# Three pairs of PSUM banks for the first round of an attention scan, and outputs of the second stream copied head by head

## The chip, the cores and the metric

The kernel runs on one core of one Trainium2 chip. The metric is the device time of one execution in microseconds (us); lower is better. Engines are named as in the profile: PE is TensorE (PEld its weight loads), DVE is VectorE, ACT is ScalarE, POOL is GpSimd and SP is SyncE, which here only issues transfers. SPq and ACTq are transfers issued from those engines' queues.

## The reference, cut to what matters

```python
def _attn_ref(r, k, v, w, u):                    # B 4, H 8, S 768, D 48
    state = zeros(B, H, D, D)
    for t in range(S):
        y[:, :, t] = r_t . (state + (u * k_t) v_t^T)
        state = w_t[:, :, :, None] * state + k_t v_t^T
x = attn.transpose(0, 2, 1, 3).reshape(B * S, H * D)     # 3072 tokens x 384
x = ((x @ w_a) * (x @ w_b)) @ w_out                      # d_ff 1536, "gated"
h = x @ w_in;  g = max(h, 0) + alpha * min(h, 0)         # d_ff 2048, "leaky"
out = g @ w_out2
```

All of it is float32. In the two feed-forward layers each factor is split in a high and a low part, and three products (high by high, high by low, low by high) are summed: lines 166 to 168 of the helper `three_products`.

## The kernel before, in words

**The scan.** Queries r, keys k and decays w lie with channels on partitions. A pair of heads is stacked at partitions 0 and 64 (48 channels each, `ROWS` = 112 rows in all), and a *unit* is such a pair in one batch. A round, called `n` or `duo` in the code, handles four units over half of the sequence (384 tokens each); they form two *streams* `j` = 0, 1 of two units. Eight rounds (`DUOS`) make the whole. Inside blocks of 64 tokens the decays are unrolled by doubling: a *leaf* step and then *levels* 1 to 5. Before level p the queries (`step_r`) and the keys (`step_k`) of each stream are multiplied by products of decays over 2^(p-1) tokens, which `products_of_w` makes; then 24 small matmuls a stream (`level`, line 696; 48 records of PE in the trace) write scores of both heads to two PSUM banks, and DVE merges them under a mask into `a_sb` (`merge_level`, line 948, one instruction a head). The leaf scores are merged by `merge_leaf` (line 938). Level 5 is copied, not merged (`copy_last_level`, one head by ACT, one by DVE). Then the keys are multiplied a last time (`last_step_k`), turned by PE (`turn_keys`, line 711), copied by ACT (`copy_kt`), multiplied with the values (`key_values`, line 725), carried through the blocks as states by DVE (`carry_states`, lines 971 and 979), and the outputs are summed: `weighted_values` (line 740) and `state_products` (line 756).

A round has 11 phases. Round 0 stands ahead of everything else and runs alone. From phase 1 of round 1 on, each phase is a slot in the loop over `g` of the gated layer (8 tiles of 384 tokens by 12 column blocks of `w_a` and `w_b`): in an iteration PE does `up_a(g)`, `down(g-1)`, `up_b(g)`, and then a phase of the scan. The leaky layer follows, without scan work.

**PSUM.** There are eight banks: `products` has five of them (numbers 0 to 4), `acc[0..2]` one each. Bank 4 is where the gated layer has its `a` product. In round 0 the gated layer doesn't run yet. The banks of a level are

```python
def level_bank(phase, hd):
    return BANK * (2 * (phase % 2) + hd)
```

so levels alternate between banks 2, 3 (odd levels) and 0, 1 (even ones), and `level` waits on PE for the merges of the level two before (`merged`). The keys of stream j are turned into banks 2j and 2j + 1, and so `turn_keys` waits for the merges of level 4, and for stream 1 for the copies of level 5 too.

**The order of the work** is written out by hand, for each engine a list, and is in order on each. In round 0 the queries and the last key step run on POOL, the other key steps and the merges on DVE; DVE's list for round 0 stands line by line at the end of its block. SP issues in its order: keys, queries and decays of round 0; the first weights (`load_piece`); the values of stream 0 and 1 (`load_v`); the queries of round 1 (`load_r`), each after the values of its own stream have landed; the keys of round 1 (`load_k`) once each stream's keys are turned; more weights; and the moves below.

**Outputs and moves.** `output_parts` lists what ACT copies out of PSUM as high parts (`copy_outputs`) and DVE subtracts for the low parts (`lower_outputs`, line 1021): stream 0 in four parts of 192 columns, stream 1 in two parts of 384 columns, both of 112 rows, where rows 48 to 63 are filler. The gated layer's input needs 128 rows: the filler rows get the fourth 16-channel pieces of a unit, which `move_rows` transfers out of `f_y` (lines 346, six of 48 KB each, `KT` = 3 by two row groups). For the first of three groups q the move waits for stream 0's parts alone, for the others for all six, since a later copy would overwrite what was moved. PE's `wait_x` asks for part 3 at kt = 0 and for all parts at kt > 0, and for the move of that kt. In round 0 ACT issues two of the six moves.

**Weights** of the gated layer come in 36 pieces through three staging buffers: SP loads, ACT splits off the high part (`split_hi`, line 138), DVE (POOL for the first five) the low part (`split_lo`, line 143). `FIRST_NEW[f]` is the first piece that is split in iteration f of the first tile; SP loads piece p + 3 into the buffer of piece p in the same iteration.

## Time and profile before

| | before |
|---|---|
| median of 3 runs | 1025.76 us (1025.4 to 1025.85) |
| profiled execution: its own time | 1024.34 us |
| its span, first to last instruction | 1022.5 us |
| PE busy | 1000.7 us, 98% of the span |
| PE idle by the stretches, 0 to 50 us | 16.8 us |
| DVE, ACT, POOL busy | 559.5, 288.7, 24.4 us |

The profiled execution lies 1.42 us under the median; 1.84 us of its time are outside of the span. A timeline row gives the start in us from the span's start, the length in us, the engine, the line, the operation with what it writes and reads, how often, and in brackets how long the engine was idle before and what ended that. The PE idle time to 50 us is the sum over stretches of length minus busy time.

### The profile page before, as it was taken

Reading aid. Unit: us, or ns where it says so; the run is one execution under the profiler, and the core shown is the slowest. Engines: PE = TensorE matmul, PEld = TensorE weight load, DVE = VectorE, ACT = ScalarE, POOL = GpSimd, SP = SyncE. Lnnn points to the kernel's source line nnn. Section 1 sums busy time; section 2 is a strip of 40 time slices with the busy share of each in tenths; the row PEclk is TensorE's granted clock in tenths of the full one; section 3 lists DMA queues with packets and bytes.
Section 4 is the critical chain, followed back from the end, with each engine's and each line's share of the span. In section 5 each row is a group of like instructions: output and inputs, shape, how many; then the busy total and the mean of one; then the engine's idle time right before and its main releaser. Section 6 shows DMA issues by size and latency. Waiting matters only on the chain.

```text
span 1022.5 us, 29089 instructions
## 1 busy us (share of the span) xinstructions
PE 1000.7 (98%) x12448; PEld 976.0 (95%) x12448; DVE 559.5 (55%) x1170; ACT 288.7 (28%) x604; POOL 24.4 (2%) x24
## 2 busy tenths in 40 slices
PE   5799999999999999999999999999999999999998
PEld 5799999999999999999999999999999999999998
DVE  7487664655656646556432437645455554545554
ACT  3435314223232242241222434222222212122212
POOL 4400000000000000000000000000000000000000
PEclk9999999999999999999999999999999999999999
DMA  6554311411213013010020313010101010101000
GB/s 159 140 156 113 87 55 30 114 29 47 69 30 91 25 30 92 15 52 25 25 60 1 114 58 124 1 47 1 47 1 47 1 46 0 46 0 47 10 15 24
DMA packets 42167, 53.01 MB, mean 52 GB/s; under 512 B 5184, under 2 KB 42048, under 8 KB 42048
## 3 DMA queue, kind: packets, MB, share of 16 engines
q1 hardware_dynamic: 40624, 51.04, 17.5%
q8 instruction: 94, 1.54, 0.6%
q10 hardware_dynamic: 1424, 0.23, 0.1%
q14 instruction: 25, 0.20, 0.1%
HBM read 39.46 MB, written 9.44 MB: 48 GB/s over the span
## 4 chain that ended last, share of the span: by engine, by line
PE 96%; DVE 1%; issue 1%; ACT 0%; DMA 0%; ACTq 0%; DVEq 0%; SPq 0%
PE products L166 18%; PE products L167 16%; PE products L168 16%; PE acc L168 12%; PE acc L166 11%; PE acc L167 11%; PE products L696 5%; PE products L711 1%; PE products L740 1%; PE products L756 1%; PE products L673 1%; PE products L725 1%; DMA x_parts<-f_y 0%; DVE k_in L931 0%; DVE a_sb L948 0%
## 5 line engine op out<-in xcount | busy, mean ns | idle before, releaser
L166 PE MATMUL products<-x_parts,weights_hi 128*128 128x384 f32 x576 | 201.0, 349 | 3.6 <-DMA x_parts<-f_y 1.5
L167 PE MATMUL products<-x_parts,weights_hi 128*128 128x384 f32 x576 | 194.2, 337 | 0.0
L168 PE MATMUL products<-x_parts,weights_lo 128*128 128x384 f32 x576 | 193.9, 337 | 0.0
L1239 DVE TENSOR_SCALAR leaky_low<-products,leaky_al 128x384 f32<-128x384 f32 x128 | 79.0, 617 | 169.6 <-PE products L168 169.5
L1099 DVE TENSOR_TENSOR g_sb<-a_g,products 128x384 f32<-128x384 f32 x96 | 53.2, 554 | 195.4 <-issue 133.1
L1186 ACT ACTIVATE leaky_g_hi<-leaky_g_sb 128x384 fp32r<-128x384 f32 x128 | 67.3, 525 | 295.0 <-DVE leaky_g_sb L1244 295.0
L514 ACT ACTIVATE g_hi<-g_sb 128x384 fp32r<-128x384 f32 x96 | 50.3, 524 | 255.0 <-DVE g_sb L1099 255.0
L166 PEld LDWEIGHTS products<-x_parts,weights_hi 128*128 128x128 f32 x576 | 108.1, 188 | 8.9 <-issue 5.0
L168 PEld LDWEIGHTS products<-x_parts,weights_lo 128*128 128x128 f32 x576 | 108.2, 188 | 0.0
L167 PEld LDWEIGHTS products<-x_parts,weights_hi 128*128 128x128 f32 x576 | 108.2, 188 | 0.0
L168 PE MATMUL acc<-g_hi,weights_lo 128*128 128x384 f32 x288 | 97.5, 338 | 0.0
L166 PE MATMUL acc<-g_hi,weights_hi 128*128 128x384 f32 x288 | 97.4, 338 | 0.0
L167 PE MATMUL acc<-g_lo,weights_hi 128*128 128x384 f32 x288 | 96.9, 336 | 0.0
L514 ACT ACTIVATE a_g<-products 128x384 f32<-128x384 f32 x96 | 47.3, 493 | 129.9 <-PE products L168 129.8
L696 PEld LDWEIGHTS products<-r_in,k_in 48*64 48x64 f32 (+1 forms) x3840 | 61.0, 139 | 13.0 <-issue 9.6
L1105 DVE TENSOR_TENSOR g_lo<-g_sb,g_hi 128x384 fp32r<-128x384 f32 x96 | 53.4, 557 | 36.3 <-ACT g_hi L514 36.1
L1226 DVE TENSOR_TENSOR leaky_g_lo<-leaky_g_sb,leaky_g_hi 128x384 fp32r<-128x384 f32 x128 | 70.3, 549 | 5.3 <-ACT leaky_g_hi L1186 4.7
L1244 DVE SCALAR_TENSOR_TENSOR leaky_g_sb<-products,leaky_low 128x384 f32<-128x384 f32 x128 | 70.4, 550 | 0.3
L696 PE MATMUL products<-r_in,k_in 48*64 48x32 f32 (+1 forms) x3840 | 65.7, 223 | 3.4 <-DVE a_sb L948 1.4
L167 PE MATMUL products<-x_parts,leaky_rest_hi 128*128 128x384 f32 x192 | 65.0, 339 | 0.0
L166 PE MATMUL products<-x_parts,leaky_rest_hi 128*128 128x384 f32 x192 | 64.9, 338 | 0.0
L168 PE MATMUL products<-x_parts,leaky_rest_lo 128*128 128x384 f32 x192 | 64.9, 338 | 0.0
(85 smaller groups left out, 1754.9 us busy)
## 6 DMA issues: line engine op xcount, KB each, us to landing
k_in<-in_k_dram SPq DMA_DIRECT2D x16, 336.0 KB, 4.2
r_in<-in_r_dram SPq DMA_DIRECT2D x16, 336.0 KB, 5.2
stage<-in_w_out_dram SPq DMA_DIRECT2D x14, 384.0 KB, 3.2
w_v<-in_v_dram SPq DMA_DIRECT2D x16, 288.0 KB, 3.8
y_dram<-x_in SPq DMA_DIRECT2D x8, 576.0 KB, 3.0
x_in<-y_dram SPq DMA_DIRECT2D x8, 576.0 KB, 4.6
out_dram<-leaky_out_sb SPq DMA_DIRECT2D x7, 576.0 KB, 3.3
stage<-in_w_dram SPq DMA_DIRECT2D x10, 336.0 KB, 3.8
```

The lines of the kernel that those rows point to most:

```text
L166: pe.matmul(out, w_hi, x_hi, start=first, stop=False)
L167: pe.matmul(out, w_hi, x_lo, start=False, stop=False)
L168: return pe.matmul(out, w_lo, x_hi, start=False, stop=last)
L514: return act.activation(out, in_, ACT.Copy)
L673: last = pe.matmul(view(tile, at + BLOCK * c, [[1, BLOCK]], BLOCK, BLOCK * par), key_blocks(k_scratch[j], hd, c, par), key_blocks(r_leaf[j ...
L696: last = pe.matmul(view(products, level_bank(phase, hd) + 32 * (CH * j + c), [[1, 32]], rows, BLOCK * par), key_blocks(k_in[j], hd, c, par ...
L1099: dve.tensor_tensor(g_sb[:, :], a_g[:, :], b_ps(g), ALU.mult).then_inc(g_ready, 1)
L1105: dve.tensor_tensor(g_lo[f % 2][:, :], g_sb[:, :], g_hi[f % 2][:, :].bitcast(F32), ALU.subtract).then_inc(g_lo_ready, 1)
L1186: return act.activation(out_, in_, ACT.Copy)
L1226: dve.tensor_tensor(self.g_lo[f % 4][:, :], self.g_sb[f % 2][:, :], self.g_hi[f % 4][:, :].bitcast(F32), ALU.subtract).then_inc(self.g_lo_ ...
L1239: dve.tensor_scalar(self.low[f % 2][:, :], h, 0.0, self.al[:, f:f + 1], ALU.min, ALU.mult).then_inc(self.low_ready, 1)
L1244: dve.scalar_tensor_tensor(self.g_sb[f % 2][:, :], h, 0.0, self.low[f % 2][:, :], ALU.max, ALU.add).then_inc(self.g_ready, 1)
```

## The change

It does five things.

1. In round 0 the levels use three pairs of banks: levels 1 and 4 have banks 2, 3, level 2 banks 0, 1, level 3 `acc[0]` and `acc[1]`, level 5 bank 4 and `acc[2]`. The keys of stream 1 are turned into `acc[0]`, `acc[1]`. PE's waits are now for merges that lie further back.
2. On DVE the key steps of a level go ahead of the merges of the levels before; the last key steps of round 0 move from POOL to DVE, and POOL waits for them before its last query steps.
3. On ACT `copy_last_level` of round 0 goes behind the copies of the turned keys.
4. SP loads the queries of round 1 after both loads of values have landed, and the second of them after the first has landed.
5. Stream 1's outputs are copied and lowered in four parts of 48 rows in every round, in place of two of 112 rows, so all six moves need stream 0's parts alone; SP issues five of them in round 0 and ACT one, ahead of the copies of stream 1. Beside this `FIRST_NEW` has one piece in iteration 1 and two in iteration 3, where there were two and one.

```diff
-OUTPUTS = 6
+OUTPUTS = 8
-FIRST_NEW = [5, 5, 7, 9, 10, 11, 13, 15, 16, 17, 18, 18, 18]
+FIRST_NEW = [5, 5, 6, 8, 10, 11, 13, 15, 16, 17, 18, 18, 18]
...
-            def level_bank(phase, hd):
-                return BANK * (2 * (phase % 2) + hd)
+            def level_ps(n, phase, hd):
+                if n == 0 and phase == 3:
+                    return acc[hd], 0
+                if n == 0 and phase == 5:
+                    return (products, 4 * BANK) if hd == 0 else (acc[2], 0)
+                return products, BANK * (2 * ((phase + (n == 0 and phase == 4)) % 2) + hd)
+
+            def keys_ps(n, j, hd):
+                return (acc[hd], 0) if n == 0 and j == 1 else (products, stream_bank(j, hd))
...
-                units_of_1 = (0, 2, hi[0:ROWS, TT:3 * TT], lo[0:ROWS, TT:3 * TT])
+                units_of_0 = [(0, ROWS, *group) for group in units_of_0]
+                units_of_1 = [(row0, D, 0, 2, hi[row0:row0 + D, TT:3 * TT], lo[row0:row0 + D, TT:3 * TT]) for row0 in (0, 64)]
...
                 def move_last_unit(n):
+                    sp.wait_ge(copied, outputs_copied(n, 3))
+                    sp.wait_ge(lowered, outputs_lowered(n, 3))
                     for q in range(KT):
-                        part = 3 if q == 0 else OUTPUTS - 1
-                        sp.wait_ge(copied, outputs_copied(n, part))
-                        sp.wait_ge(lowered, outputs_lowered(n, part))
-                        for row0 in ((0, 64) if n > 0 or q == 0 else (0,)):
+                        for row0 in ((0, 64) if n > 0 or q < KT - 1 else (0,)):
                             move_rows(sp, n, q, row0)
...
-                                if n == 0:
-                                    sp.wait_ge(v_loaded[j], 16)
+                                if n == 0 and j == 0:
+                                    sp.wait_ge(v_loaded[0], 16)
+                                    sp.wait_ge(v_loaded[1], 16)
+                                elif n == 0:
+                                    sp.wait_ge(r_loaded[2], 16)
                                 load_r(n + 1, j)
...
                         if step == 6:
-                            last_step_k(0, j)
+                            pool.wait_ge(k_last[1], 1)
...
-                    if phase == 6:
+                    if phase == 6 and n > 0:
                         copy_last_level(n)
                     elif phase == 7:
                         copy_kt(n, 0)
                         copy_kt(n, 1)
+                        if n == 0:
+                            copy_last_level(n)
                     elif phase == 10:
                         copy_outputs(n, 0)
                         if n == 0:
                             shared.split_hi(act, BETWEEN_OUTPUTS)
+                            act.wait_ge(lowered, outputs_lowered(n, 3))
+                            move_rows(act, n, KT - 1, 64)
                         copy_outputs(n, 1)
-                        if n == 0:
-                            act.wait_ge(lowered, outputs_lowered(n, OUTPUTS - 1))
-                            for q in range(1, KT):
-                                move_rows(act, n, q, 64)
...
                     h = 1 << phase
-                    if phase >= 3:
+                    if n == 0:
+                        if 2 <= phase <= 4:
+                            pe.wait_ge(merged, (merges(0, 0, 1), merges(0, 0, 3), merges(0, 1, 1))[phase - 2])
+                    elif phase >= 3:
                         pe.wait_ge(merged, merges(n, phase - 2, 1))
...
                 def turn_keys(n, j):
-                    if j == 0:
+                    if n == 0:
+                        pe.wait_ge(merged, merges(0, 2 + j, 1))
+                    elif j == 0:
                         pe.wait_ge(merged, merges(n, 4, 1))
...
                 def key_values(n, j):
                     pe.wait_ge(copied, copies(n, "keys", j, 1))
+                    if n == 0 and j == 1:
+                        pe.wait_ge(merged, merges(0, 4, 1))
...
+                step_k(0, 1, 1)
                 merge_leaf(0, 1)
-                step_k(0, 1, 1)
                 step_k(0, 0, 2)
+                step_k(0, 1, 2)
+                products_of_w(0, 0, 2, (3,))
                 merge_level(0, 0, 1)
                 merge_level(0, 1, 1)
...
```

The semaphore arithmetic (`copies`, the parts in `lower_outputs`) follows these and is left out. What the lists become on DVE in round 0 (line numbers shift: `step_k`, 931, is 947 now, `merge_level`, 948, is 965, and 1012 is `last_step_k`), from the merges of level 2 on:

```order
L948 COPY_PREDICATED a_sb<-level_mask,products 128x96x4 [waits merged,masks_loaded,products_done1] x2
L931 TENSOR_TENSOR k_in0<-k_in0,f_y 112x48x8 [waits products_done0,k_stepped0,f_done]
L948 COPY_PREDICATED a_sb<-level_mask,products 128x48x8 [waits merged,masks_loaded,products_done1]
L931 TENSOR_TENSOR k_in1<-k_in1,f_y 112x48x8 [waits products_done1,k_stepped1,f_done]
L948 COPY_PREDICATED a_sb<-level_mask,products 128x48x8 [waits merged,masks_loaded,products_done1]
L931 TENSOR_TENSOR k_in0<-k_in0,f_y 112x24x16 [waits products_done0,k_stepped0,f_done]
L948 COPY_PREDICATED a_sb<-level_mask,products 128x24x16 [waits merged,masks_loaded,products_done1]
L931 TENSOR_TENSOR k_in1<-k_in1,f_y 112x24x16 [waits products_done1,k_stepped1,f_done]
L948 COPY_PREDICATED a_sb<-level_mask,products 128x24x16 [waits merged,masks_loaded,products_done1]
```

This was before; the same engine and place with the change:

```order
L965 COPY_PREDICATED a_sb<-level_mask,products 128x96x4 [waits merged,masks_loaded,products_done1] x2
L947 TENSOR_TENSOR k_in0<-k_in0,f_y 112x24x16 [waits products_done0,k_stepped0,f_done]
L947 TENSOR_TENSOR k_in1<-k_in1,f_y 112x24x16 [waits products_done1,k_stepped1,f_done]
L965 COPY_PREDICATED a_sb<-level_mask,acc0 128x48x8 [waits merged,masks_loaded,products_done1]
L1012 TENSOR_TENSOR k_in0<-k_in0,f_y 112x12x32 [waits products_done0,k_stepped0,f_done]
L1012 TENSOR_TENSOR k_in1<-k_in1,f_y 112x12x32 [waits products_done1,k_stepped1,f_done]
L965 COPY_PREDICATED a_sb<-level_mask,acc1 128x48x8 [waits merged,masks_loaded,products_done1]
L965 COPY_PREDICATED a_sb<-level_mask,products 128x24x16 [waits merged,masks_loaded,products_done1] x2
```

The key steps of level 3 (48x8) now stand ahead of level 2's merges (96x4), and both last key steps stand between the merges of level 3.

On SP, the loads of round 1's queries and what stands around them, before:

```order
L350 DMA w_v<-in_v_dram 128x2x288 [waits k_first0,f_done,r_stepped0,staged1]
L350 DMA w_v<-in_v_dram 128x2x288 [waits k_first1,f_done,r_stepped1,staged2]
L350 DMA r_in<-in_r_dram 112x2x384 [waits v_loaded0]
L350 DMA r_in<-in_r_dram 112x2x384 [waits v_loaded1]
L350 DMA k_in<-in_k_dram 112x2x384 [waits products_done0]
L350 DMA k_in<-in_k_dram 112x2x384 [waits products_done1]
```

and with the change:

```order
L361 DMA w_v<-in_v_dram 128x2x288 [waits k_first0,f_done,r_stepped0,staged1]
L361 DMA w_v<-in_v_dram 128x2x288 [waits k_first1,f_done,r_stepped1,staged2]
L361 DMA r_in<-in_r_dram 112x2x384 [waits v_loaded1,v_loaded0]
L361 DMA r_in<-in_r_dram 112x2x384 [waits r_loaded2]
L361 DMA k_in<-in_k_dram 112x2x384 [waits products_done0]
L361 DMA k_in<-in_k_dram 112x2x384 [waits products_done1]
```

The order is the same; the two waits moved.

## Rows read from the trace of the kernel before

**Rows 1.** The page, part 1: busy us (share of the span) and instructions.
```profile
PE 1000.7 (98%) x12448; PEld 976.0 (95%) x12448; DVE 559.5 (55%) x1170; ACT 288.7 (28%) x604; POOL 24.4 (2%) x24
```
**Rows 2.** Windows: stretch, length, busy us (records) by engine, granted clock, DMA share, GB/s.
```profile
8.00:20.00 12.00, 9.38 (x326) 8.87 (x323) 10.26 (x16) 3.83 (x8) 6.57 (x6) 1.00 0.51 127
20.00:30.00 10.00, 7.22 (x285) 6.68 (x281) 7.27 (x14) 2.20 (x4) 7.58 (x9) 1.00 0.58 154
40.00:50.00 10.00, 8.15 (x204) 7.30 (x201) 4.38 (x11) 3.92 (x9) 3.66 (x2) 1.00 0.47 122
100.00:200.00 100.00, 99.78 (x1809) 95.33 (x1807) 60.51 (x143) 30.29 (x70) 0.00 (x0) 1.00 0.25 67
```
**Rows 3.** The chain of waits from 0 to 52 us: start, length, what.
```profile
28.32 2.32 issue
...
44.13 2.99 DMA x_parts<-f_y
```
**Rows 4.** Timeline of PE in round 0 and behind it.
```profile
19.01 2.79 PE L696 MATMUL products<-r_in,k_in 48*64 48x32 f32 x96 [1.36 <-DVE a_sb L948]
...
26.55 0.87 PE L696 MATMUL products<-r_in,k_in 48*32 48x32 f32 x48 [0.49 <-DVE k_in L931]
27.34 0.98 PE L711 MATMUL products<-ident,k_in 48*64 48x48 f32 x25
30.64 2.15 PE L711 MATMUL products<-ident,k_in 48*64 48x48 f32 x69 [2.32 <-issue]
...
36.23 1.53 PE L740 MATMUL products<-a_sb,w_v 64*48 64x64 f32 x48 [0.79 <-DVE state L979]
...
54.57 1.60 PE L696 MATMUL products<-r_in,k_in 48*64 48x32 f32 x96
```
**Rows 5.** DMA queues from 24 to 28 us, then from 28 to 30: packets, MB, share.
```profile
q1 hardware_dynamic: 459, 0.66, 65.0%
...
q8 instruction: 1, 0.02, 3.6%
```
**Rows 6.** Timeline of SP: the loads of round 1's queries.
```profile
24.32 1.05 SPq L350 DMA_DIRECT2D r_in<-in_r_dram  x2
```
**Rows 7.** Timeline of DVE, then POOL, in round 0.
```profile
17.11 1.85 DVE L948 COPY_PREDICATED a_sb<-level_mask,products 128x384 f32<-128x384 int32 x2
22.40 0.89 DVE L931 TENSOR_TENSOR k_in<-k_in,f_y 112x384 f32<-112x384 f32 x1
...
22.00 0.87 POOL L490 TENSOR_TENSOR r_in<-r_in,f_y 112x384 f32<-112x384 f32 x1 [0.41 <-PE products L696]
```
**Rows 8.** Timelines of PE, SP and DVE at the end of round 0.
```profile
44.84 0.42 PE L166 MATMUL products<-x_parts,weights_hi 128*128 128x384 f32 x1 [0.36 <-DMA x_parts<-f_y]
47.26 0.41 PE L166 MATMUL products<-x_parts,weights_hi 128*128 128x384 f32 x1 [1.13 <-DMA x_parts<-f_y]
...
41.80 4.24 SPq L346 DMA_DIRECT2D x_parts<-f_y  x4
...
43.03 1.02 DVE L1021 TENSOR_TENSOR x_parts<-products,x_parts 112x384 fp32r<-112x384 f32 x2 [1.31 <-ACT x_parts L514]
43.97 1.04 DVE L938 COPY_PREDICATED a_sb<-leaf_mask,products 128x384 f32<-128x384 int32 x2
```
**Rows 9.** Timelines of ACT and PE behind the outputs of round 3.
```profile
246.17 1.11 ACT L514 ACTIVATE x_parts<-products 112x192 fp32r<-112x192 f32 x3
247.23 0.49 ACT L514 ACTIVATE a_g<-products 128x384 f32<-128x384 f32 x1
...
248.62 0.33 PE L166 MATMUL products<-x_parts,weights_hi 128*128 128x384 f32 x1
```
**Rows 10.** Timelines of PE, DVE, SP and ACT in the gated layer's iterations 1 to 4.
```profile
63.03 0.41 PE L166 MATMUL products<-x_parts,weights_hi 128*128 128x384 f32 x1 [0.41 <-DVE g_sb L1099]
...
60.60 1.82 DVE L143 TENSOR_TENSOR weights_lo<-stage,weights_hi 128x768 fp32r<-128x768 f32 x2
...
67.27 3.49 SPq L133 DMA_DIRECT2D stage<-in_w_b_dram  x6
...
71.65 0.49 ACT L514 ACTIVATE a_g<-products 128x384 f32<-128x384 f32 x1 [1.40 <-PE products L168]
```

52 lines of the change are left out of this document (32 added, 20 removed).

## The prediction

> **What bounds the kernel now.** I began with the page's busy times: PE is busy for 98% of the span [rows 1]. The windows say where the missing 2% lie. From 100 to 200 us PE idles for 0.22 us; up to 50 us it idles for 16.8 us (the table above), 7.25 of them in the three stretches before 50 us [rows 2], where the granted clock reads 1.00 throughout. So only the scan's round 0 and the first iterations of the gated layer have time to give; behind them anything that the change does can only keep PE waiting. The chain of waits up to 52 us names two large single pieces [rows 3]: 2.32 us of "issue" at 28.32, and 2.99 us for a move into `x_parts` that ends at 47.13. Beside these, the levels leave small gaps of 0.4 to 1.6 us, which end with a merge or a key step of DVE [rows 4].
>
> **The gap at 28.32** stands within `turn_keys` of stream 0: 25 records of 48, then nothing, then the other 23 in one go with stream 1's 48 [rows 4]. No semaphore lies between them. What the trace has there is the DMA queues' share [rows 5]: from 24 to 28 us the DMA engines carry 0.66 MB, 65% busy, for the loads of round 1's queries, which SP issued from 24.32 on [rows 6], and no instruction packet; between 28 and 30 us there is one packet of 0.02 MB on q8, the queue of instructions. I read this as PE running out of instructions, since the fetch of the next block stood behind the query loads. The Trainium skill (Runtime: NRT & Kernel Launch, "Instruction fetch mechanics") says that instructions come in blocks of 16 KiB through a DMA queue of the engine's own, and that the cost of a block is mostly hidden; q8's packet has that size, the 2.32 us contradict "hidden" for this place. By that sentence the gap would have another cause and stay; this is the second rival.
>
> **The change, step by step.**
>
> *Loads of the queries (SP).* The first now waits for both loads of values. Stream 1's query load of before, which waited for the second load of values, was the second of the two issues [rows 6] and began near 25.05, so the first load is issued some 0.7 us later, and its packets run from about 26 instead of 25.3. PE leaves level 4 near 24.4 and needs the new block at the 26th record of `turn_keys`, 28.1. If the fetch is asked for near 25.4 it is ahead of the packets now. Gain 2.32, with 0 as the other bound. I take 2.32, since the second query load can't stand in the way: it waits for the first one's landing, near 28.7. What is queued behind it on SP are the key loads of round 1. Those are issued only once keys are turned, so they lose nothing, but the three loads now go out within about 1.5 us.
>
> *Levels (PE, DVE).* Level 3 on PE started at 19.01, released by a merge [rows 4]. Now it needs only the leaf's merges, and can start when level 2 of stream 1 ends, near 17.5: 1.5 us earlier. Little of this lives until the turn. DVE was busy for 10.26 of 12 us and 7.27 of 10 [rows 2], and it has the same instructions to do, with one key step more (0.56, from POOL) and three merges fewer (0.56 each) ahead of the first turned keys; the two merges of level 1 take 1.85 [rows 7] and now stand ahead of level 3's key steps. POOL works beside it, and a DVE step with two SBUF inputs that meets POOL's takes 0.89 instead of 0.56 [rows 7]: key steps that are released by the same matmuls as POOL's query steps meet them always. Walking the list with these lengths I get level 4 at 21.6 to 22.2, level 5 at 24.9, and the turn at 27.1 instead of 27.34. Gain 0.25; bounds -0.4 (each meeting lost) and 1.5 (level 3's lead kept).
>
> *Behind the turn.* From the break's end to `weighted_values` of stream 0 it took 5.59 us (30.64 to 36.23) [rows 4]: turned keys, ACT's copies, products, ten state steps. The same instructions stay on this path. ACT's copy of level 5, 0.97 long, leaves it and hides beside the key-value products; level 3's second merge must now be done before stream 1's keys turn, near 28.3, just in time. So `weighted_values` start near 33.7.
>
> *The next blocks of instructions.* The three loads that now leave close together are 1 MB; at the pace of before (0.66 MB in 65% of 4 us, 0.25 MB a us [rows 5]) they run from 30 to 34 while PE needs further blocks. I charge 0.2 us; bounds 0 and 0.85 (a fetch that starts only when the last key load is through).
>
> *Moves (SP, ACT, PE).* PE waited 1.13 us at 47.26 for the second group's move [rows 8], 1.29 us start to start beyond a matmul's 0.18. All moves now go out from 41.80 on, where SP's four took 4.24 including its wait for stream 1 [rows 8]; five at about 0.65 end near 45, so the second group lands near 46.4, in time. But DVE has two more subtractions of 0.47 ahead of the leaf merges, which started at 43.97 [rows 8]: the first ends near 45.9, and PE's first `w_b` product waits for it, with 45.36 as the time that it had. Of the 15 matmuls behind it the last starts near 48.45 instead of 49.26. Gain 0.8; bounds 0 (ACT's move issue, 0.7 long, holds its copies, or the fifth move is late) and 1.3. Cover for the rest: the low parts of stream 1 are wanted only at the second group.
>
> *Outputs in rounds 1 to 7.* ACT has two more copies, DVE two more subtractions (2 x 0.5, hidden: DVE is busy for 60.5 of 100 us there [rows 2]). ACT's three copies took 1.06 until `a_g` [rows 9], one of them half as long: 0.40 for a full one. So `a_g` ends at 247.72 + 0.8 = 248.5, and `up_b`, whose first matmul ran at 248.62 [rows 9], wants its weights one matmul ahead, at 248.45, and waits for `a_g`. Each round then loses 0.1 to 0.2 with the weight load that no longer hides; in six rounds, since round 7's `up_b` doesn't wait for this. Loss 0.7; bounds 0 and 1.5.
>
> *`FIRST_NEW`.* PE waited 0.41 at 63.03 for `g_sb` [rows 10], which stood behind DVE's two splits at 60.60, 1.82 long; with one split it doesn't. Gain 0.5. But piece 9 is now loaded in iteration 2, at the place of before's piece 10 (SP from 67.27, 3.49 long [rows 10], and landed, I estimate, near 72.4; all of it some 0.9 earlier now), and split by ACT, 0.8 long, in iteration 3 ahead of `a_g`, which ran at 71.65 [rows 10]. The split would end near 72.3 and hold `up_b(4)` for 0.5. Together 0; bounds 0.7 either way.
>
> **Sum.** 2.32 + 0.25 - 0.2 + 0.8 - 0.7 + 0 = 2.5 us less. Against the profiled execution: 1024.34 - 2.5 = 1021.8. The median of the runs lies 1.42 us higher, so the predicted time is 1025.76 - 2.5 = 1023.3 us.
>
> **Rivals.**
>
> *A, a different start of the faster pace (chance 0.10).* 96 records of a level took 2.79 us at 19.01 and 1.60 at 54.57 [rows 4], with the granted clock given as 1.00, that is 2.4 GHz, in both [rows 2]. The pace changes somewhere between. If fewer breaks bring this forward by about 3 us of small matmuls, twice the length of `weighted_values` of one stream (1.53 [rows 4]), it gives 3 x (1 - 1.60 / 2.79) = 1.3 us more: 1022.0. Against it: the levels keep their breaks. The Trainium skill (TensorE: Matmul & The Clock Gate, "Part 1: The HAM clock gate") has PE at half its rate until it has been active for a while; the pace agrees, the granted clock of the rows doesn't show it.
>
> *B, the gap stays (0.25).* Either the fetch is late for another reason or it now waits behind the first query load, which was delayed by less than the fetch needs. Then the keys go on near 30.6 to 31.3, and the keys' part of the sum is 0 to -0.7 in place of 2.32 + 0.25, and with 0.8 - 0.7 the total is 0.1 faster to 0.6 slower: 1025.7 to 1026.4. For it: PE comes to level 4's end earlier, if at all, by a few tenths only.
>
> *C, a fetch behind three loads (0.05), the case of slower.* The second query load and both key loads are now issued within 1.5 us. If PE asks for its next block after the second load's packets have begun, at 30, instead of before, that block waits for 1 MB and for some 0.3 MB of weights behind it, at 0.25 MB a us until about 35.2. PE goes on 2.5 us after that (before: from the end of the query loads near 28.1 to 30.64), in `key_values` of stream 1, at 37.7. `weighted_values` would begin near 38.6, 2.4 later than before, and with 0.8 - 0.7 the whole would be 2.3 slower: 1028.1. It decides whether the first turn is reached before or behind the second query load's issue at 28.7; I put it at 28.1 plus 1, which is close. Against it: in the chain of before no second piece of issue comes near 2.32 us, though the key loads ran there too.
>
> *D, the sum holds in sign but is eaten (0.15)*: outputs 1.5, `FIRST_NEW` 0.7 and the next blocks 0.85 at their bad ends give 2.32 + 0.25 + 0.8 - 1.5 - 0.7 - 0.85 = 0.3: 1025.4.
>
> **How the numbers follow.** My forecast has 0.45. A measurement of this kernel can tell about 0.2%, 2.05 us, from no change, so faster means below 1023.7. Forecast and A give faster in most of their cases (0.51 of 0.55), and a lucky part of the others adds 0.03: 0.54. Within 0.2% lie most of B and D and the rest of the forecast: 0.40. Slower is C with a part of B at its bad end: 0.06. The range goes from 1020.9 (2.32, levels 0.8, moves 1.1, A's 1.3, less 0.7 for outputs: 4.8) to 1025.9, within B; outside are C, the worse part of B and little below. The likeliest case alone spans 1021.9 to 1024.3.
>
> **What would show it.** The turn of both streams in one piece of 96 records; the q8 packet between 24.5 and 27 us instead of behind 28; `weighted_values` near 33.7; level 3 at 17.5 but level 5 not before 24.8; no wait for a move at the second group, but one of 0.6 us for `a_sb` in the first; `up_b` behind each round's outputs 0.1 to 0.2 late; the wait before `up_a(3)` gone and one before `up_b(4)` instead. It is wrong if a gap ended by "issue" with more than 1 us stands anywhere from 27 to 40 us, or if the idle time of PE behind 60 us grows by over 2 us.

## The result, and the profile after

The changed kernel takes 1027.93 us (median of 20 runs) against 1024.43 us for the kernel before (20 runs beside them on the same chip): ratio 1.0038, 95% interval 1.0029 to 1.0047, so 3.9 us slower by the ratio (the two medians are 3.5 us apart). The profiled execution has a time of 1027.83 us and a span of 1026.0 us, against 1022.5 us [rows 1]. The page, part 1, of the changed kernel:

```profile
PE 1002.9 (98%) x12448; PEld 975.8 (95%) x12448; DVE 572.7 (56%) x1188; ACT 297.0 (29%) x620; POOL 23.4 (2%) x22
```

PE is busy 2.2 us longer with the same number of matmuls, DVE 13.2 us and ACT 8.3 us longer. Where the time went is best read by setting the two lists of PE's matmuls beside each other, since there are 12448 in both: the start of the n-th in the changed kernel minus the start of the n-th before (worked out from the trace's single records).

| matmul no. | what it stands behind | before, us | difference, us |
|---|---|---|---|
| 900 | last state products of round 0 | 40.99 | -3.86 |
| 1200 | the first up products | 59.53 | -0.67 |
| 2000 | iterations 1 to 4 of the gated layer | 104.69 | -0.39 |
| 9200 | outputs of rounds 1 to 6 | 501.0 | +1.89 |
| 9700 | round 7 and its outputs | 539.3 | +3.59 |
| 12200 | nearly all | 976.1 | +3.51 |

So a lead of 3.9 us was there when the kernel before was at 41 us; 3.2 of it are gone 18 us later; 2.3 us are then lost behind the outputs of six rounds, and 1.7 in and behind the seventh.

**The head.** PE's timeline of the changed kernel from level 4 of round 0 to the first up product (start, length, line, tiles, shape, count, idle time before and what ended it):

```profile
22.39 2.78 PE L707 MATMUL products<-r_in,k_in 48*64 48x32 f32 x96 [1.63 <-DVE k_in L947]
...
27.44 1.53 PE L725 MATMUL products<-ident,k_in 48*64 48x48 f32 x48
28.78 1.53 PE L725 MATMUL acc<-ident,k_in 48*64 48x48 f32 x48
...
33.75 0.89 PE L756 MATMUL products<-a_sb,w_v 64*48 64x64 f32 x48 [1.64 <-DVE state L997]
...
42.62 0.66 PE L166 MATMUL products<-x_parts,weights_hi 128*128 128x384 f32 x1 [0.94 <-DMA x_parts<-f_y]
```

The keys of both streams turn in one piece, without the 2.32 us of "issue" [rows 4], and `weighted_values` begin 2.48 us before [rows 4]. The `weighted_values` also run at another pace: 48 of them in 0.89 us where they took 1.53 [rows 4]. The DMA queues from 24 to 28 us of the changed kernel (packets, MB, share of 16 engines) now hold the instruction packet, at 25.03 us, and less data [rows 5]:

```profile
q1 hardware_dynamic: 280, 0.38, 32.0%
q8 instruction: 1, 0.02, 1.7%
```

**The granted clock.** Windows of the changed kernel, with the columns of [rows 2]:

```profile
31.70:41.90 10.20, 6.69 (x307) 5.96 (x299) 6.66 (x28) 9.15 (x23) 5.40 (x4) 1.00 0.52 138
41.90:48.70 6.80, 6.06 (x18) 5.48 (x18) 2.67 (x6) 0.82 (x2) 1.84 (x1) 0.50 0.74 201
48.80:60.00 11.20, 11.20 (x150) 10.59 (x150) 10.04 (x21) 2.72 (x5) 0.00 (x0) 1.00 0.77 166
```

From 41.9 to 48.7 us the granted clock is 0.50, the 1.2 GHz level, and it's just there that the 18 first up products run, 0.32 us from start to start. In the kernel before the same stretch is at 1.00:

```profile
31.70:41.10 9.40, 8.26 (x276) 7.90 (x270) 4.81 (x24) 7.14 (x21) 3.09 (x2) 1.00 0.65 162
41.10:48.70 7.60, 5.81 (x161) 5.28 (x154) 3.54 (x9) 2.33 (x4) 3.50 (x2) 1.00 0.36 87
```

and the products stand 0.17 us apart. At 0.32 instead of 0.17 us, 18 products take 2.6 us longer. The trace of before has no entry of the clock ahead of 41.1 us, that of the changed kernel none ahead of 31.7; a window that starts earlier shows 1.00 as well, though the small matmuls there have the slower pace. So a stretch's 1.00 means something from a trace's first entry on only, and that first entry agrees with the change of pace of `weighted_values`.

**The moves of round 0.** The low clock isn't all that takes the lead. At the first up product it is down from 3.9 to 2.2 us already (42.62 against 44.84 [rows 8]), since PE waits there for the first moves. SP issued these late. DVE's and SP's timelines of the changed kernel:

```profile
38.12 0.35 DVE L1039 TENSOR_TENSOR x_parts<-products,x_parts 112x192 fp32r<-112x192 f32 x1
```

```profile
35.70 3.71 SPq L133 DMA_DIRECT2D stage<-in_w_b_dram  x6
39.51 3.29 SPq L357 DMA_DIRECT2D x_parts<-f_y  x5
```

Stream 0's low parts were done at 38.47, but SP was still issuing pieces of weights until 39.41, and the first of its moves left 1.04 us after the parts that it needs. In the kernel before, DVE was done with them at 41.72 and the move left at 41.80 [rows 8]:

```profile
41.37 0.35 DVE L1021 TENSOR_TENSOR x_parts<-products,x_parts 112x192 fp32r<-112x192 f32 x1
```

PE's break of 1.16 us of "issue" ahead of 40.52 ends before the moves land, so it costs nothing beside this.

**The rounds behind.** ACT's outputs of round 3 and the next `a_g`, to be read beside [rows 9], in the changed kernel:

```profile
246.46 2.22 ACT L520 ACTIVATE x_parts<-products 112x192 fp32r<-112x192 f32 x5
248.71 0.49 ACT L520 ACTIVATE a_g<-products 128x384 f32<-128x384 f32 x1
```

and PE's `up_b` behind it:

```profile
249.25 0.44 PE L166 MATMUL products<-x_parts,weights_hi 128*128 128x384 f32 x1 [0.17 <-ACT a_g L520]
```

From the start of the group to `a_g` it is 2.25 us where it was 1.06 [rows 9]. The group of five holds one copy of 112x192, with 0.21 us to the next, and four of 48x384: 0.51 us each from start to start, though one alone is only 0.48 long. Before, a copy of 112x384 stood 0.37 from a copy like it and was 0.52 long. PE's start to start across this place is 0.51 us in place of 0.17 (from 248.74 to 249.25), and the product behind it starts another 0.11 us late: 0.45 us in this round, 0.38 us on average over rounds 1 to 6 (2.28 / 6).

In round 7 it is more. PE's waits of the changed kernel from 480 us to the end (line, whose result, us in all, times, longest), of which only the last line is there before:

```profile
PE products L166 <- DVE x_parts L1039: 1.1, 1, 1.1
PE products L166 <- DVE g_sb L1129: 0.5, 1, 0.5
PE products L166 <- issue: 0.3, 1, 0.3
```

and DVE there, in the changed kernel:

```profile
524.76 2.74 DVE L1039 TENSOR_TENSOR x_parts<-products,x_parts 112x192 fp32r<-112x192 f32 x5
```

against 1.28 us for three before. No round follows, so the banks of `products` go over to the up products: `up_b` waits for all of `lowered`, and DVE's last subtraction ends at 527.5 us: 1.42 us from matmul to matmul (526.23 to 527.65), a loss of 1.33. The wait of 0.5 us for `g_sb`, at 509.8, is another matter: DVE stood in "issue" ahead of it, with nothing of the outputs near, and it costs 0.38. `g_sb` started 0.46 us after the end of the product that it reads, where 0.09 is usual. The kernel before has such starts too (0.45 us, at 243.7 and 350.5 us), but PE waits for none of them there.

**`FIRST_NEW`.** The wait at 63.03 [rows 10] is gone. There is one before `up_b(4)`, behind a split of a piece that ACT waited for, PE's and then ACT's timeline of the changed kernel:

```profile
72.50 0.44 PE L166 MATMUL products<-x_parts,weights_hi 128*128 128x384 f32 x1 [0.73 <-ACT a_g L520]
```

```profile
71.22 0.85 ACT L138 ACTIVATE weights_hi<-stage 128x768 fp32r<-128x768 f32 x1 [2.41 <-DMA stage<-in_w_a_dram]
71.97 0.47 ACT L520 ACTIVATE a_g<-products 128x384 f32<-128x384 f32 x1
```

By the differences between matmuls, 0.77 us are won at the one place and 0.99 lost at the other: 0.2 us lost.

### The profile page after: what moved, and what is told of

It is laid out like the page before. It is cut to its first block and busy times, and to the rows that moved or that the text cites. A ratio compares the mean times of both kernels' runs of the same rounds, so it can differ in the third digit from the quotient of the medians.

```text
span 1026.0 us, 29108 instructions
## 1 busy us (share of the span) xinstructions
PE 1002.9 (98%) x12448; PEld 975.8 (95%) x12448; DVE 572.7 (56%) x1188; ACT 297.0 (29%) x620; POOL 23.4 (2%) x22
## 3 DMA queue, kind: packets, MB, share of 16 engines
q1 hardware_dynamic: 40672, 51.09, 17.5%
## 5 line engine op out<-in xcount | busy, mean ns | idle before, releaser
L707 PEld LDWEIGHTS products<-r_in,k_in 48*64 48x64 f32 (+1 forms) x3696 | 58.2, 137 | 12.3 <-issue 11.3
L707 PE MATMUL products<-r_in,k_in 48*64 48x32 f32 (+1 forms) x3696 | 62.8, 221 | 2.8 <-DVE k_in L947 2.0
```

The lines of the kernel that those rows point to most:

```text
L707: last = pe.matmul(view(tile, at + 32 * (CH * j + c), [[1, 32]], rows, BLOCK * par), key_blocks(k_in[j], hd, c, par, rows), queries, start ...
```

## The experiments

Theory 1: the split by head costs 0.4 us a round and 1.3 to 1.7 in round 7. Theory 2: PE's breaks between 38 and 42.6 us bring the clock down, and this takes the head's lead. Each ratio is to runs of the kernel before taken beside it, with its 95% interval.

### 1. The split in round 0 alone

```diff
-hi[row0:row0 + D, TT:3 * TT], ...) for row0 in (0, 64)]
+hi[row0:row0 + rows, TT:3 * TT], ...) for row0, rows in (((0, D), (64, D)) if n == 0 else ((0, ROWS),))]
```

with the counts of `copied` and `lowered` by round, and the moves of q = 1, 2 behind all parts from round 1 on.

> The changed kernel with the second stream's outputs copied by head in round 0 only; from round 1 on they are two parts of 112 rows, and the moves of q = 1, 2 wait for them, as before. Theory 1 (the loss is the split: four copies of 48 rows, about 0.4 us in each of rounds 1 to 6, and 0.37 + 1.33 us around round 7): some 4.1 us less than the changed kernel, so about 0.6 us less than the kernel before, ratio 0.999 to 1.000; the breaks of TensorE ahead of the weight products of rounds 1 to 6 (0.3 us each) and the break of 1.24 us after round 7 gone. Theory 2 (the low clock at the first up products takes the head's lead, 3.2 us): says nothing on rounds 1 to 7, the clock falls here too, at about 42 us; with it alone as the cause the ratio would stay at 1.0035. Rival (the loss in rounds 1 to 7 is another order of the weights' pieces): the ratio stays at 1.0035.

Measured: 1.0010 (1.0001 to 1.0019). The span is 1022.3 us. ACT behind round 1's outputs in this kernel:

```profile
108.30 1.11 ACT L532 ACTIVATE x_parts<-products 112x192 fp32r<-112x192 f32 x3
109.42 0.49 ACT L532 ACTIVATE a_g<-products 128x384 f32<-128x384 f32 x1
```

Against before, matmul 2000 stands at -0.28 us and 12200 at -0.23: nothing is lost in rounds 1 to 7. Theory 1 holds for rounds 1 to 7, in place and size (3.9 us are lost in the changed kernel between the same two matmuls). The time itself missed: 0.999 to 1.000 was expected, and of the head only 0.3 us was left in the trace. PE still stopped for 1.99 us of "issue" in the turn. The clock didn't fall in this trace, against the expectation; of its 11 runs 8 have a mean clock below 1.000.

### 2. Outputs and moves as before in every round

```diff
-OUTPUTS = 8
+OUTPUTS = 6
```

with `output_parts`, the moves and DVE's wait as before.

> The changed kernel with outputs and moves as before in every round, round 0 too; levels, loads and FIRST_NEW as changed. Theory 1: as the run with the split in round 0 alone, plus what the earlier moves were worth there (0 to 1.3 us): ratio 0.999 to 1.001. Theory 2: if the break before the first up products is what brings the clock down, it is as long here or longer, and the clock is at half from about 42 us again; the ratio then is 1.000. If it stays at 1.0, the ratio is 0.996 to 0.997.

Measured: 1.0003 (0.9993 to 1.0013), the time of before. In the trace nothing is lost between matmuls 2000 and 9700 (0.02 us). The clock fell for 3.4 us, from 46.1 on, over ten of the first up products.

### 3. The split alone

The kernel before with the same `output_parts`, moves and `OUTPUTS = 8` as the changed one.

> The kernel before with the outputs by head and the moves that need the first stream's alone, and nothing else. Theory 1: 2.4 us for rounds 1 to 6 and 1.7 us for round 7, less 0 to 0.8 us of the earlier moves in round 0: slower by 3.3 to 4.1 us, ratio 1.0032 to 1.0040. Rival (the split costs what the prediction gave it, 0.7 us, less 0.8 us of the moves): ratio 1.000. Theory 2: the clock from 41 us on as in the kernel before, at 1.0.

Measured: 1.0057 (1.0043 to 1.0071), more than expected. The trace accounts for 2.41 us between matmuls 2000 and 9200 and 1.33 to 9700, and the wait for `g_sb` isn't there. At matmul 2000 it is 0.42 us behind the kernel before, and 4 of its 5 runs have a mean clock below 1.000. The moves did land earlier: the first up product starts at 44.28 and the second group at 46.83, which were 44.84 and 47.26 [rows 8]. But from 45.6 to 49.0 us the clock was low, and the last product of the first up products starts at 49.74, 0.5 us later than before.

### 4. Filled breaks

```diff
+def fill(count):
+    for _ in range(count):
+        pe.matmul(view(acc[2], 0, [[1, D]], D, 0), ident[0:D, :], ident[0:D, :], start=True, stop=True)
```

called with 70 ahead of `leaf(1, 0)` and with 60 ahead of `first_ups`.

> The changed kernel with matmuls of 48 columns that nothing reads put into TensorE's two breaks between 38.3 and 42.6 us: 70 ahead of round 1's leaf products and 60 ahead of the first up products, about as long as the breaks of 1.35 and 1.13 us. Theory 2 (the breaks bring the clock down): it stays at 1.0 there, the first up products run at the pace of 0.17 us, and the kernel takes about 3 us less than the changed one, ratio to the kernel before 1.0000 to 1.0010. Rival 1 (the clock falls by something else, such as the earlier start of the full pace): the clock falls at about 42 us all the same, and the time is the changed kernel's or up to 1 us more, ratio 1.0035 to 1.0045. Rival 2 (the low clock is made good later, since the up products wait for pieces anyway): the clock stays up and the time does not change.

Measured: 1.0203 (1.0189 to 1.0216), 20.5 us slower; no theory had this. The fills took far longer than the breaks. PE's timeline of this kernel:

```profile
39.66 6.84 PE L672 MATMUL acc<-ident 48*48 48x48 f32 x136
...
48.97 9.80 PE L672 MATMUL acc<-ident 48*48 48x48 f32 x120
```

(Two records each, as every matmul on small tiles here.) The records are 0.045 us from start to start, and 0.080 at the low clock, where those of the turned keys, also 48 columns wide, are 0.028 us apart at the slow pace (48 between 27.44 and 28.78 above), and other small ones 0.017 at the fast (96 in 1.60 [rows 4]). The turned keys go to the four quarters of the array in turn; the fills all use the same rows and columns. The Trainium skill (TensorE: Matmul & The Clock Gate, "Part 3: Packing small matmuls — row/col tiling") has small matmuls run at the same time when they are placed on different tiles of the array; the rows agree, as the records spread over four parts are nearly three times as close as those of the fills. The fills differ in one thing more: all of them write the same columns of one bank. No run tells the two apart.

The run tests theory 2 all the same. Windows of this kernel:

```profile
39.70:45.10 5.40, 5.40 (x130) 5.40 (x123) 2.22 (x4) 2.79 (x5) 3.51 (x2) 1.00 0.31 59
45.20:58.60 13.40, 13.40 (x234) 13.40 (x232) 2.09 (x4) 0.00 (x0) 0.00 (x0) 0.50 0.56 142
58.70:62.10 3.40, 3.40 (x12) 3.40 (x12) 0.00 (x0) 0.00 (x0) 0.00 (x0) 0.50 0.00 0
62.30:70.00 7.70, 7.65 (x127) 7.08 (x126) 5.45 (x13) 1.51 (x3) 0.00 (x0) 1.00 0.08 12
```

PE is busy without a break from 39.7 us, and the clock still falls to 0.50 near 45.1, stays there through 13.4 us of unbroken small matmuls, and rises only behind the first wide ones (128 rows, 384 columns), which begin at 58.7. So the clock can fall without a break, and theory 2 has lost its cause. But the fills changed the kind of work as well as the breaks, and so the run doesn't show what brought the clock down in the changed kernel. That it falls there, and that it costs, stands.

### 5. The loads alone

```diff
-if n == 0:
-    sp.wait_ge(v_loaded[j], 16)
+if n == 0 and j == 0:
+    sp.wait_ge(v_loaded[0], 16)
+    sp.wait_ge(v_loaded[1], 16)
+elif n == 0:
+    sp.wait_ge(r_loaded[2], 16)
```

> The kernel before with the waits of the two loads of r for round 1 as in the changed kernel, and nothing else. The prediction's own step (the load queue leaves the instruction block room, the break of 2.32 us inside turn_keys goes): 2.3 us faster, ratio 0.9978. Rival, formed on the runs so far (the time at which the block is fetched differs from run to run, its break was 1.0 to 2.6 us in four traces, and a kernel whose full pace starts early falls back to the low clock for 3 to 7 us around 42 to 49 us and gives about 1.5 us back): ratio 0.9990 to 1.0005, and more of the runs with a mean clock of 0.998 than in the kernel before.

Measured: 0.9995 (0.9986 to 1.0004), by the rival; the prediction's 0.9978 is outside. The break inside the turn is near 0.1 us, and matmul 2000 stands at -1.50 us in the trace; but 3 of 12 runs, not more than before, have a mean clock below 1.000.

### 6. The levels alone

The changed kernel less parts 4 and 5, `FIRST_NEW` included.

> The changed kernel with outputs, moves, the waits of the r loads and FIRST_NEW of the kernel before: only the levels of round 0 through three pairs of banks and the order of VectorE are left of the change. Prediction's step: 0.25 us faster, 0.9998, with the break inside turn_keys as in the kernel before. Theory of the eaten lead: levels 3 ends earlier, but levels 4 and 5 wait for the key steps, and weighted_values starts within 0.3 us of the time before; ratio 0.9995 to 1.0010.

Measured: 0.9992 (0.9981 to 1.0003), a little under both expectations, which its interval holds. The theory of the eaten lead missed: `weighted_values` start at 34.32, 1.9 us before those of the kernel before and not within 0.3. The trace's break inside the turn is 1.21 us of "issue", not 2.32, without any change to the loads, and its matmul 2000 stands at -2.72 us, the best head of all.

### 7. Levels and loads

The changed kernel with `output_parts`, moves and `FIRST_NEW` as before.

> The changed kernel with outputs, moves and FIRST_NEW of the kernel before: levels and r loads are left of the change. By the prediction's sum 2.6 us faster, 0.9975. By the theory that the lead is given back at the low clock and differs from run to run: within 0.1% of the kernel before, 0.9990 to 1.0005; runs whose mean clock is 1.000 some 1.5 us shorter than those at 0.998. Beside the run with whole outputs (1.0003) it tells what FIRST_NEW costs: 0 to 0.3 us.

Measured: 0.9990 (0.9981 to 0.9999). The prediction's 0.9975 is outside. Only 1 of its 12 runs has a mean clock below 1.000.

### 8. `FIRST_NEW` alone

```diff
-FIRST_NEW = [5, 5, 7, 9, 10, ...
+FIRST_NEW = [5, 5, 6, 8, 10, ...
```

> The kernel before with FIRST_NEW as changed and nothing else. The traces of the two kernels say: the break before up_a(3) (0.6 + 0.2 us) goes and one of 0.9 us before up_b(4) comes, the sum +0.2 us: ratio 1.0002, and the first difference after 76 us at most 0.3 us. The prediction set this at 0 with 0.7 us either way. Rival (the early piece also delays a transfer that is waited for): 0.5 us and more.

Measured: 1.0002 (0.9992 to 1.0011), too coarse to tell 0.2 us from nothing, but not 0.5. In the trace the difference between matmuls 1300 and 1500 grows by 0.16 us. Its head shows how far one execution is from another: the program is that of before up to 60 us, but PE's stop of 2.3 us came in another place,

```profile
27.07 1.23 PE L696 MATMUL products<-r_in,k_in 48*64 48x32 f32 x54 [2.33 <-issue]
```

which is in level 4, and matmul 2000 stands 2.1 us later than before.

### 9. By-head copies ordered by rows

```diff
+if len(parts) == 8:
+    parts[5], parts[6] = parts[6], parts[5]
```

> The changed kernel with the middle two of the four by-head copies swapped, so that two copies of rows 0 to 47 follow each other and then two of rows 64 to 111 (VectorE's too): same instructions, one change of rows instead of three. Theory 1a (a copy that starts at other rows than the one before it doesn't overlap it: 0.50 us from start to start, against 0.37 us): the copies start 0.37, 0.50, 0.37 us apart, ScalarE is free 0.26 us earlier, TensorE's break ahead of the weight products of rounds 1 to 6 falls from about 0.3 to at most 0.1 us, and the kernel is 1.5 us faster than the changed one: ratio to the kernel before 1.0020 to 1.0025. Theory 1b (copies of 48 rows never overlap): 0.50 us each as before, ratio 1.0035.

Measured: 1.0020 (1.0008 to 1.0033), as 1a has it. The interval touches that of the changed kernel (from 1.0029), so the step between the two rests on the traces. ACT's group of round 1 in this kernel is 0.27 us shorter than 2.22:

```profile
107.53 1.95 ACT L522 ACTIVATE x_parts<-products 112x192 fp32r<-112x192 f32 x5
```

and between matmuls 2000 and 9200 the loss is 0.77 us instead of 2.28. In round 7 PE waits 0.71 us for DVE instead of 1.1. Single records of the four copies in this kernel settle it: they start 0.37, 0.51 and 0.39 us apart, and only the middle pair changes its first row. It's the change of the first row from one copy to the next that keeps them from overlapping. The by-rows kernel still loses 0.13 us a round (0.77 / 6).

### 10. Four copies cut by columns

```diff
-units_of_1 = (0, 2, hi[0:ROWS, TT:3 * TT], ...)
+units_of_1 = [(unit, 1, *[x[0:ROWS, TT * (1 + unit):TT * (2 + unit)] for x in (hi, lo)]) for unit in range(2)]
```

> Levels and r loads as changed, FIRST_NEW as before, and the second stream's outputs in every round in four copies too, but cut by columns: 112 rows by 192 columns each, the moves after the last. Theory 1 (a copy costs by its columns and by the change of rows, not by being one more): 0.21 us from start to start, four of them 0.86 us where two of 384 columns took 0.90 us, no breaks in rounds 1 to 7, ratio as for levels and loads alone, 0.9985 to 1.0000. Rival (four copies in place of two are what costs): 0.3 us or more a round, ratio 1.0015 or above.

Measured: 1.0007 (0.9997 to 1.0017), above the first's range and below the rival's. ACT's group of round 1 in this kernel:

```profile
108.59 1.22 ACT L520 ACTIVATE x_parts<-products 112x192 fp32r<-112x192 f32 x5
```

Five copies in 1.22 us, where the by-head ones needed 2.22; the loss between matmuls 2000 and 9200 is 0.00. So two copies more cost nothing in themselves; cutting by rows instead of columns is the whole 0.38 us a round. It costs twice: a copy of 48 rows and 384 columns takes as long as one of 112 rows, so four of them are twice the work, and three of them change the first row. The wait for `g_sb` near 508 is there (0.38). What lifts the ratio beside it is probably the head: 9 of its 12 runs have a mean clock below 1.000.

### 11. A try at both gains

The kernel of experiment 1, with the order of experiment 9 in round 0 and `FIRST_NEW` as before.

> Meant to beat both: levels, r loads and the moves that need the first stream's outputs alone as changed, the split by head in round 0 only and there ordered by rows, FIRST_NEW as before. If the earlier moves are worth the prediction's 0.8 us and the 0.26 us of the row order come on top: ratio 0.9980 to 0.9985, under levels and loads alone (0.9990). If the split in round 0 makes the clock fall back more often (25 of 36 runs with it, 31 of 115 without, about 1.5 us each time): no gain on levels and loads alone, 0.9990 to 1.0000, with more runs at a mean clock of 0.998.

Measured: 1.0001 (0.9990 to 1.0012), no gain. This trace has the largest lead of all at matmul 900, 4.48 us, and none at 2000: 0.71 us behind the kernel before. PE waits for the moves, and then the products run at the low clock (0.57 over 42 to 49 us). PE's timeline of this kernel, and SP's:

```profile
44.34 0.66 PE L167 MATMUL products<-x_parts,weights_hi 128*128 128x384 f32 x1 [3.49 <-DMA x_parts<-f_y]
```

```profile
35.92 4.10 SPq L134 DMA_DIRECT2D stage<-in_w_b_dram  x6
40.13 4.21 SPq L370 DMA_DIRECT2D x_parts<-f_y  x5
```

DVE had stream 0's low parts done at 38.47 here too; SP's first move left 1.66 us later, behind the weights, and the second, at 40.92, took 3.3 us to land.

### 12. Levels and loads once more

> The kernel of levels_and_loads once more, to have it beside these three and to see a second trace of it: ratio 0.9980 to 1.0000 if its 0.9990 holds. The theory that the time of the instruction blocks differs from run to run expects another break inside the levels or turn_keys than the 1.22 us at 27.28 us, by up to 1.5 us, and the same times from start to start from 110 us on, within 0.1 us.

Measured: 0.9998 (0.9989 to 1.0008). The 0.9990 wasn't confirmed; taken together the two say 0.0 to 1 us faster, which is no difference by this kernel's measurement. The break inside the turn, in the kernel's first trace,

```profile
28.52 0.78 PE L727 MATMUL products<-ident,k_in 48*64 48x48 f32 x20 [0.94 <-issue]
```

and in its second:

```profile
29.41 0.87 PE L727 MATMUL products<-ident,k_in 48*64 48x48 f32 x21 [1.05 <-issue]
```

One program, and all of it comes 0.8 to 0.9 us later here, and 1.1 us later at matmul 900. Yet both traces have matmul 2000 at -1.04 us: in the first PE waited three times for moves of round 0 (0.24, 0.92 and 0.84 us), in the second once (1.09 us).

## What the traces say together

Each row is one profiled execution; differences to before in us, worked out from single records.

| kernel | "issue" in the turn | first clock entry | low clock | no. 900 | no. 2000 | 2000 to 9200 | 9200 to 9700 |
|---|---|---|---|---|---|---|---|
| before | 2.32 | 41.1 | none | 0 | 0 | 0 | 0 |
| changed | none | 31.7 | 6.8 us | -3.86 | -0.39 | +2.28 | +1.70 |
| split in round 0 (1) | 1.99 | 41.0 | none | -0.77 | -0.28 | -0.01 | 0.00 |
| outputs as before (2) | 0.71 | 35.9 | 3.4 us | -2.25 | +0.38 | -0.02 | +0.04 |
| split alone (3) | 0.95 | 38.7 | 3.4 us | -1.51 | +0.42 | +2.41 | +1.33 |
| loads alone (5) | near 0.1 | 39.3 | none | -1.69 | -1.50 | 0.00 | 0.00 |
| levels alone (6) | 1.21 | 39.3 | none | -2.14 | -2.72 | 0.00 | +0.02 |
| levels, loads (7) | 0.94 | 38.8 | none | -2.34 | -1.04 | -0.02 | 0.00 |
| by rows (9) | none | 38.2 | 3.4 us | -2.86 | -1.04 | +0.77 | +1.31 |
| quarters (10) | none | 36.8 | 3.4 us | -3.47 | +0.02 | 0.00 | +0.36 |
| both gains (11) | none | 32.7 | 6.8 us | -4.48 | +0.71 | -0.11 | +0.02 |
| levels, loads (12) | 1.05 | 40.0 | none | -1.23 | -1.04 | -0.06 | -0.01 |

Three readings. The two columns on the right go by the output copies: nothing with those of before or with quarters, 2.3 to 2.4 and 1.3 us with those by head, 0.8 and 0.9 with those ordered by rows, and 0.4 us more around 508 us in the three kernels of the table that have both eight parts in every round and the changed list of DVE. The lead at no. 900 isn't what is left at no. 2000: the four kernels with 2.8 us or more keep between 1.0 and -0.7. And with 14 traces (experiments 4 and 8 among them, 38.3 with a fall and 41.6 without), the clock fell again in all seven that rose by 38.75 us, and in none of the seven that rose from 38.8 on. Seven against seven is an observation, not a cause.

The breaks of "issue" bear on the prediction's reading of the 2.32 us. Between 20 and 48 us PE has 29 of them of 0.3 us or more in the 14 traces, and 28 end 2.3 to 2.9 us after the last packet on q8 began, that of before among them (28.05 and 30.64). That is strong evidence that PE waited there for a block of instructions. Why the packet comes when it does is another question.

What the low clock is worth can be read from the changed kernel's own 20 runs: 7 with a mean granted clock of 1.000 have a median of 1027.2 us, 13 with 0.997 or 0.998 one of 1028.6. That is 1.4 us, in 13 of 20 runs here and in 28 of 91 of the kernel before that ran beside the experiments, where the two medians are 1.4 us apart too.

## Why the prediction was wrong

It forecast 2.5 us less and gave a slower result by more than 0.2% a chance of 0.06; 3.9 us more were measured. By its own steps:

- **Outputs in rounds 1 to 7: the step that failed.** It set 0.7 us, with 1.5 as the bound; the traces have 4.0 us in the changed kernel and 3.7 in the split alone, between matmuls 2000 and 9700, and experiment 1 takes all of it back. The size of a copy was read from a group of mixed shapes (1.06 us for three) as 0.40 from start to start, and carried over to copies that start on other rows. The new ones need 0.51. `a_g` came 1.19 us later after the group's start, not 0.8, and with 0.38 us instead of 0.1 to 0.2 on PE, times six, that is 2.3 us. Experiments 9 and 10 show why: a copy that starts on other rows than the one before doesn't overlap it. Where the row changes once among the four copies, `a_g` comes 0.91 us later and the loss is 0.13 a round, as forecast for 0.8: the step from ACT to PE was right, and the 0.40 was the term that failed.
- A rule for this was to be had. The Trainium skill (VectorE: DVE Perf Modes, "Two Vector instructions with no wait between them") holds a VectorE instruction back until the earlier ones are finished if its inputs or its output start in another quadrant, a group of 32 partitions, than the last ones did. DVE's subtractions agree: 0.58 us from start to start and 0.55 long, where 112-row ones stood 0.47 apart. By that rule four by-head subtractions are 2.3 us in place of 0.9. ACT's rows show the same behaviour.
- **"Round 7's `up_b` doesn't wait for this".** It waits: 1.1 us for DVE's last subtraction, since behind the last round the banks are handed to the up products, and together with the 0.38 us at `g_sb` that makes 1.7 us. The wait stands in the code (`step_at(g) is None`), and wasn't costed.
- **Loads.** Right in the profiled execution: the packet at 25.03 us (forecast 24.5 to 27), both streams turned in one piece, `weighted_values` at 33.75 (33.7). Wrong as an expectation: 2.32 us was one execution's break. The four traces with the old waits have 2.32, 0.95, 1.21 and (experiment 8) 0.18 there, with 2.33 in another place; the ten with the new ones 0 to 1.99. Alone the loads are worth 0.5 us, give or take 0.9. The mechanism is half settled: PE waited for a block of instructions, but that the query loads alone held its packet back isn't shown. Experiment 1 has the new waits and the same 0.38 MB from 24 to 28 us, and its packet came at 27.51 us, with a stop of 1.99. Rival B ("the gap stays") has a share in it.
- **Levels.** 0.25 was forecast; level 3 started near 17.5 as said, level 4 at 22.39, level 5 at 25.5 and the turn at 27.44, 0.1 us after that of before. Nothing in this execution, 0.8 us give or take 1.1 when alone.
- **Moves.** 0.8 was forecast. The wait for the second group is gone, and yet the last of the first up products starts at 48.56 instead of 49.26, with round 0 3.9 us ahead. The low clock (2.6 us, less the 1.1 us of wait that is gone) and the moves took the rest, 1.6 us ahead of the first up product. "All moves now go out from 41.80 on" took SP as free; with round 0 ahead, it still had weights to issue. Experiment 11 shows this at its largest.
- **Rival A** named an earlier rise of the pace and gave it 1.3 us. The rise came, 9.4 us earlier. That the clock could fall again was in no case of the prediction.
- **`FIRST_NEW`**: 0 was forecast, with 0.5 each way; 0.77 and 0.99 were measured, a loss of 0.2.

Of the prediction's two signs of being wrong one came: PE's idle time behind 60 us grew from 5.0 to 7.6 us, by more than 2. The other is on the edge: the 1.16 us of "issue" began at 39.36 and ended at 40.52.

Together, for the profiled execution: -3.9 (head) + 3.2 (low clock and moves) + 0.3 (to matmul 2000, `FIRST_NEW` in it) + 2.3 + 1.7 - 0.1 = +3.5 us.

**What stays open.** What sets the moment at which a block of instructions is fetched, which differs by up to 2.8 us between executions of the same instructions, and what makes the clock fall between 42 and 47 us: the runs only rule out that breaks of PE are needed for it. Why DVE stands in "issue" ahead of `g_sb` at 509 us wasn't tried, nor were moves issued ahead of the weights. Whether levels and loads alone are faster at all isn't settled: 0.9990 and 0.9998.

## What to carry to other kernels

A cost read from a group of instructions holds for their shape and their place alone: before an operation is split, look at start to start of single ones, cut it by columns rather than rows, and keep neighbours on ACT and DVE on the same first row. A cost that recurs in every round outweighs one in the prologue: 0.4 us times six and a last round that is wired differently were worth more than the largest gap of the head. And a stall without a semaphore ("issue") that one trace shows is a draw: see it in a second trace before its full length goes into a sum.

## What the runs showed of the hardware

- Copies and subtractions of 48 rows take about as long as those of 112 (0.48 against 0.52 us on ACT, 0.55 for both on DVE, for 384 columns), and with a change of the first row between 0 and 64 they don't overlap: 0.51 instead of 0.37 us from start to start on ACT, 0.58 instead of 0.47 on DVE.
- Records of 48x48 matmuls on the same part of the array, all into the same columns of PSUM, stand 0.045 us apart at the 2.4 GHz level and 0.080 at 1.2 GHz; small ones spread over four parts, 0.017 and 0.028.
- The granted clock fell to 0.50 while PE was busy for 100% of the time with such matmuls, and rose 3.4 us after wide ones began.
- The same instructions stop in "issue" in different places in two executions: 2.32 us in the turn of the kernel before, 2.33 in level 4 and 0.18 in the turn of `FIRST_NEW` alone. In 28 of 29 such breaks PE goes on 2.3 to 2.9 us after a packet of 16 KB began on the instruction queue.
